# A home of its own for the last batch's turned x2 tiles, and vector and pool work reordered in the second token mixing

## The reference

```python
# layer 1: attention without softmax, then an RMS norm
kv = einsum('bhsd,bhse->bhde', k, v); out = einsum('bhsd,bhde->bhse', q, kv)
x = out / sqrt(mean(out*out) + 1e-6) * g_norm
# layer 2 (w_tok_r, w_tok_i: 576x576; w_theta, w_ch: 512x512)
theta = x @ w_theta
y = einsum('ts,bsd->btd', w_tok_r, x*cos(theta)) + einsum('ts,bsd->btd', w_tok_i, x*sin(theta))
u = x + y; x2 = u + maximum(u @ w_ch, 0)
# layer 3 (w_tok1: 576x256, w_tok2: 256x576, w_ch1: 512x1536, w_ch2: 1536x512)
h = maximum(x2.T @ w_tok1, 0) @ w_tok2        # token mixing, the stage changed
u2 = x2 + h.T
out = u2 + maximum(u2 @ w_ch1, 0) @ w_ch2
```

## Time and profile before

| | before |
|---|---|
| median of the runs | 1263.39 us (1263.16 to 1264.73) |
| time of the profiled execution | 1261.56 us |
| its span, first to last instruction | 1259.7 us |
| mean granted TensorE clock | 0.984 |
| PE busy | 1195.4 us, 95% |
| DVE, ACT, POOL busy | 817.6, 503.4, 367.7 us |

### The profile page before, as it was taken

How to read it: one execution, slowest core, us unless ns; L and a number is a source line. 1 busy time by engine, 2 the same in 40 slices (tenths; PEclk the granted TensorE clock), 3 DMA queues, 4 the chain that set the end, 5 groups by cost and what they waited for, 6 DMA issues and landing times.

```text
span 1259.7 us, 20594 instructions
## 1 busy us (share of the span) xinstructions
PE 1195.4 (95%) x7590; PEld 1157.5 (92%) x7590; DVE 817.6 (65%) x1220; ACT 503.4 (40%) x796; POOL 367.7 (29%) x216
## 2 busy tenths in 40 slices
PE   6999999999999999987789999999999889999998
PEld 5899999999899999987777999999999889999998
DVE  3866767676767666764465566767675676666664
ACT  3533324242524333331333345555566443333331
POOL 4443435444442535240462132133022320000000
PEclk9999999999999999999889999999999999999999
DMA  9924444362715430327768487757649999999982
GB/s 256 172 40 99 76 103 84 77 111 37 149 38 111 71 80 0 76 78 229 228 219 302 158 306 294 259 228 269 254 196 346 348 326 297 257 256 286 275 200 51
DMA packets 348428, 228.12 MB, mean 181 GB/s; under 512 B 268880, under 2 KB 316368, under 8 KB 347344
## 3 DMA queue, kind: packets, MB, share of 16 engines
q1 hardware_dynamic: 348368, 227.32, 62.8%
HBM read 136.84 MB, written 92.80 MB: 182 GB/s over the span
## 4 chain that ended last, share of the span: by engine, by line
PE 61%; issue 14%; DVE 8%; POOL 5%; SPq 4%; DMA 4%; ACT 3%; DVEq 0%; POOLq 0%; ACTq 0%
PE bank L42 11%; PE bank L44 10%; PE bank L43 10%; PE bank L1196 9%; PE bank L1198 9%; PE bank L1197 9%; PE bank L252 2%; DVE weights_fraction L621 1%; POOL z_z L797 1%; SPq L154 1%; DVE tokens_cos L618 1%; DMA weights_down<-w_scratch 1%; SPq L179 1%; PE bank L240 1%; POOL z_z L799 1%
## 5 line engine op out<-in xcount | busy, mean ns | idle before, releaser
L42 PE MATMUL bank<-weights_tok,z_z 128*128 128x288 f32 x576 | 175.3, 304 | 14.7 <-ACT z_z L471 9.2
L43 PE MATMUL bank<-weights_tok,z_z 128*128 128x288 f32 x576 | 171.0, 297 | 0.0
L44 PE MATMUL bank<-weights_tok,z_z 128*128 128x288 f32 x576 | 170.9, 297 | 0.0
L42 PEld LDWEIGHTS bank<-weights_tok,z_z 128*128 128x128 f32 x576 | 109.4, 190 | 18.1 <-ACT z_z L471 10.6
L43 PEld LDWEIGHTS bank<-weights_tok,z_z 128*128 128x128 f32 x576 | 109.6, 190 | 0.0
L44 PEld LDWEIGHTS bank<-weights_tok,z_z 128*128 128x128 f32 x576 | 109.3, 190 | 0.0
L782 POOL TENSOR_TENSOR weights_rms_inverse<-weights_mean_squares,weights_minus_half 128x8 f32<-128x8 f32 x40 | 65.5, 1637 | 136.9 <-DVE weights_mean_squares L588 136.7
L797 POOL TENSOR_TENSOR z_z<-tokens_cos,z_z 128x512 fp32r<-128x512 f32 x32 | 51.3, 1604 | 177.8 <-ACT z_z L471 177.0
L478 ACT ACTIVATE weights_x_channel_major<-attention_u 128x288 fp32r<-128x288 f32 x64 | 28.4, 444 | 150.9 <-DVE attention_u L650 150.9
L42 PE MATMUL bank<-weights_x_channel_major,weights_ch 128*128 128x288 f32 x256 | 77.2, 301 | 0.0
L43 PE MATMUL bank<-weights_x_channel_major,weights_ch 128*128 128x288 f32 x256 | 75.4, 294 | 0.0
(11 more groups left out here) (271 smaller groups left out, 3700.3 us busy)
## 6 DMA issues: line engine op xcount, KB each, us to landing
g_scratch<-attention_staged SPq DMA_DIRECT2D x36, 960.0 KB, 4.7
weights_g<-g_scratch SPq DMA_DIRECT2D x24, 1152.0 KB, 8.4
g_scratch<-attention_staged SPq DMA_DIRECT2D x36, 384.0 KB, 4.7
x_scratch<-attention_u SPq DMA_DIRECT2D x8, 1152.0 KB, 4.5
x_tokens_scratch<-z_x_turned SPq DMA_DIRECT2D x128, 72.0 KB, 2.0
u_scratch<-attention_u SPq DMA_DIRECT2D x8, 1152.0 KB, 7.9
weights_raw_u<-u_scratch SPq DMA_DIRECT2D x6, 1536.0 KB, 9.1
qkv_u_left<-u_scratch SPq DMA_DIRECT2D x12, 768.0 KB, 9.8
```

What stands on the lines that cost most here:

```text
L42: eng.matmul(out, w[0], x[0], start=first, stop=False)
L43: eng.matmul(out, w[0], x[1], start=False, stop=False)
L44: return eng.matmul(out, w[1], x[0], start=False, stop=last)
```

## The change

Three edits, all about phase B.

1. The last batch's turned tiles get tiles of their own, `x2_turned_last`, behind `x2_first_tokens` in region `weights`. `turn_x2` and `store` take the tiles as an argument. ACT's wait for `prev["turned"]` moves from ahead of all its phase-B work to ahead of the first `up_hi`, which writes into region `weights`; POOL's own wait for it goes.
2. DVE's order in each batch: the two `hidden_lo` first, and then the three `x_lo` pieces ahead of residuals 0, 2 and 4.
3. POOL forms the sum `up_sum` before the third `up_lo`, not after it.

```diff
-    turned = m["x2_turned"]
+    turned, turned_last = m["x2_turned"], m["x2_turned_last"]
...
-        store(B - 1)
+        store(B - 1, turned_last)
...
-                    turn_x2(b, g - NC - 1)
+                    turn_x2(b, g - NC - 1, turned if more else turned_last)
...
-        act.wait_ge(*prev["turned"])
...
             if n == 0:
                 act.wait_ge(d_xlo, NPX)
+                act.wait_ge(*prev["turned"])
...
         def batch(n, i, pair, more=True):
-            if more:
-                x_lo(dve, n + 1, 0)
             for mt in range(NM):
                 hidden_lo(n, mt)
-            if more:
-                for piece in range(1, NPX):
-                    x_lo(dve, n + 1, piece)
             for g in range(NG):
+                if more and g % 2 == 0 and g // 2 < NPX:
+                    x_lo(dve, n + 1, g // 2)
                 residual(n, i, pair, g)
...
-        for step in range(3):
+        for step in range(2):
             up_lo(step)
         gp.wait_ge(s_up[2], DMA)
-        gp.wait_ge(*prev["turned"])
         add(up_sum, a11, a21, ALU.subtract)
+        up_lo(2)
         up_lo(3)
...
-                        [("x2_first_tokens", [P, NT, DM], F32)],
+                        [("x2_first_tokens", [P, NT, DM], F32), ("x2_turned_last", [P, 2, S], F32),
+                         ("x2_turned_last", [P, 2, S], F32)],
```

More of the change, by code:

```diff
@@ L166, in load_q, with store @@
                 load_tile(qin, q, n, j, s_q)
-        def store(n):
+        def store(n, tiles=turned):
             wait(sp, d_x2, NG * (n + 1))
@@ L171, in store, with store_turned @@
             for c in range(NC):
-                store_turned(n, c)
-        def store_turned(n, c):
+                store_turned(n, c, tiles[c // 2])
+        def store_turned(n, c, tile):
             sp.wait_ge(d_turned, NC * n + c + 1)
@@ L179, in store_turned @@
                 sp.dma_start(x2t_dram[n, :, first:first + SIDE].rearrange("(b s) d -> s b d", s=SIDE),
-                             turned[c // 2][part * SIDE:(part + 1) * SIDE, c % 2, :].rearrange("p (b d) -> p b d", d=SIDE)
+                             tile[part * SIDE:(part + 1) * SIDE, c % 2, :].rearrange("p (b d) -> p b d", d=SIDE)
                              ).then_inc(s_turned, DMA)
@@ L664, in relu_add, with turn_x2 @@
                                      op0=ALU.max, op1=ALU.add).then_inc(d_x2, 1)
-        def turn_x2(b, c):
+        def turn_x2(b, c, tiles):
             dve.wait_ge(d_x2, NG * b + NC + c + 1)
@@ L672, in turn_x2 @@
                 dve.wait_ge(p_tok, NG * (b + 1))
-            dve.transpose(turned[c // 2][:, c % 2, :], u[:, c, :]).then_inc(d_turned, 1)
+            dve.transpose(tiles[c // 2][:, c % 2, :], u[:, c, :]).then_inc(d_turned, 1)
         def tok_weight_lo(i):
@@ L770, in body @@
                     x_lo(b + 1, j)
-            turn_x2(b, NC - 1)
+            turn_x2(b, NC - 1, turned if more else turned_last)
         body(0, first=True)
```

## The result

The changed kernel takes 1283.03 us (median of 4 runs, 1280.04 to 1284.26), the kernel before 1263.28 us in the same comparison: a ratio of 1.0153, 95% interval 1.013 to 1.0176. It is 19.8 us slower. The forecast was 1279.

A forecast was written before the change was run, and what follows sets the result against it. PE, busy 95%, was taken as the bound, with phase B's one-buffer tokens loop nearly as long as its floor. The start, intervals and POOL turns put the last `mix` 15.9 us later: 1279 us, range 1264 to 1288.

The forecast's parts named there:

- The start, -9.8 us: Phase B's first `mix`: own tiles free ACT, DVE's plain x2 store wait comes next; 596.4, 9.8 us earlier.
- The first interval, 18.2: From `mix(0)` to `mix(1)`: batch 2's tokens, behind two raw weight quarters, come at 612.2; 18.2 us, 14.3 before.
- The loop, 16.2 us without POOL: Tokens' buffer, per batch: 7.2 issue to use, 2.4 to `mix`, 6.6 to next issue; exceeds PE's 12.8 by 3.4.
- the 1.5 for the low clock of the first `mix`: `mix(0)` starting on the low clock delays batch 2's token issue; between nothing and 2.4 us, 1.5 taken.
- POOL against DVE, 5.0 us in batches 1 to 3: `x_lo` 1 waits 2.3 us and `x_lo` 2 2.7 us for whole POOL instructions; batch 4 has one wait, 2.3.
- The last two intervals: The end of phase B: 16.2 us for the loop without POOL, then 12.8 us, PE's own work.
- The sum: Phase B's last `mix` at 725.7 us against 709.8, 15.9 us later; profiled execution 1277.5, median 1279.
- A slowdown by a factor of 2.8: Other reading of stretched `x_lo`: slower while POOL runs, 2.2 us at seven meetings, 15.4 us against the lock's 17.3.
- Only the loop: Rival: phase B's loop lengthens without turns between POOL and DVE; 1262 to 1274 us, chance 0.15.
- the rival of a lesser start: Rival: another wait holds `mix(0)` near 603; up to 6 us over the forecast, 1285, chance 0.12.
- The hidden loop: Rival: phase B's later tokens' load is still in time, as ACT needs it after PE's `hidden`; 1252, chance 0.08.
- POOL's sum first: Ahead of the third `mix`: removes ACT's 7.09 us wait for `up_sum` and PE's 4.72 us stall.

The follow-up runs named there:

- e1: The kernel before with the new DVE order alone; 1293.15 us, ratio 1.0228.
- e2: The changed kernel with the DVE order of before, own tiles and POOL's sum first kept; 1256.93 us, ratio 0.9946 to the kernel before.
- e6: The changed kernel with POOL's `up_lo` of steps 2 to 6 waiting for the last `x_lo` of the same batch; 1273.61 us.
- e7: The changed kernel with 24 matmuls that nobody reads ahead of `mix` in batches 0 to 6; 1277.02 us.
- e4: The kernel before with POOL's sum ahead of the third `up_lo` alone; 1262.65 us, ratio 0.9986.
- e3: The kernel before with the own tiles and the moved ACT wait alone; 1256.96 us, ratio 0.9947.
- e5: The changed kernel, but DVE does all `x_lo` after `hidden_lo` and ahead of all residuals; 1270.27 us, ratio 1.0045 to the kernel before.
- e12: The changed kernel with all `x_lo` ahead of residuals, POOL waiting for the last `x_lo`, and batch 2's tokens issued ahead of two raw quarters; 1251.49 us.

## Why the prediction was right

*The start, -9.8 us.* Right: 599.30 - 589.80 = 9.5 us after the phase's first matmul, against 19.4 before: -9.9. DVE was released by the plain x2 store, as predicted (598.46).

*The first interval, 18.2.* It was 20.1. The tokens were issued 8.1 us after `mix`, as worked out. They took 9.6 us to use and not 7.7. Of these 1.9 us 1.2 are the raw quarters ahead of them, issued 16.0 and not 14.8 us into the phase, as the 16 stores of the turned tiles took 15.6 us to issue and not 14.5; the rest is open.

*The loop, 16.2 us without POOL.* Its terms hold: 2.4 from tokens to `mix` in every batch, 6.7 to 7.4 from issue to use. That 2.4 and the 1.5 for the low clock of the first `mix` (4.65 against 3.15 us to the first residual) came out to the tenth is luck: each was picked between two bounds that no row narrowed. Where POOL has no work the interval was 17.0 (batch 5): 1.3 more for the half clock, 0.5 less for the load. e1 and e2 show that the DVE order alone makes the loss, e6 that the turns with POOL are a part of it. The part of the clock is read from rows and not isolated by a run.

*POOL against DVE, 5.0 us in batches 1 to 3.* The sum was nearly right, its parts were not. I had two meetings per batch, 2.3 and 2.7 us, and no clock. There was one, `x_lo` 2, for 2.5 us, and half clock for 2.0 (5.2 against 3.15 to the first residual): 4.5 in all. But the two are not independent. What sets the interval is when POOL's second instruction ends, and this I had at 10.9 us after `mix`; it was 10.55 (650.26 - 639.71). Until then a slow clock and a wait for POOL exchange one for one, which is the reason I gave for leaving the clock out, and e7 bears it out: on the full clock there were two meetings and the interval was no shorter. In batch 4 I had one meeting of 2.3 us; there it was 0.2 (1.42 instead of 1.22) and the half clock 1.8, again an exchange: 18.2 against 18.5.

*The last two intervals.* 16.2 and 12.8 were forecast, 17.0 and 14.1 came: a pause of 2.74 us ahead of batch 6 was enough for a first matmul at 0.58 us there, 1.3 us that the sum did not have.

*The sum.* Phase B: 15.9 later by the forecast, 17.9 by the trace (730.63 - 589.80 against 709.80 - 586.82). The medians say 19.8. The errors are +1.9 in the first interval, -2.0 in the next four and +2.1 in the last two. Two of them cancel, and that the total is as near as 4 us to the forecast is luck to this extent; the loop that outgrew PE's work is not.

The Trainium skill, page "SBUF — State Buffer", section "Who interferes with whom", says that a vector instruction with at most one SBUF input, outside the 2-port modes, does not contend with GpSimd, and that one with two contends with a GpSimd instruction that reads SBUF. The trace agrees: two residuals at 644.94 took 0.82 us with POOL's `up_lo` running to 645.72, while the `x_lo` at 647.65 stood until POOL's next one ended. A slowdown by a factor of 2.8, the other reading that the prediction weighed, does not fit: that `x_lo` took 4.6 times its 0.69 us, and the one at 645.67, which came first, its usual 1.22, while POOL's sum beside it took 4.58 instead of 3.4.

*The rivals.* "Only the loop" is nearly what e6 makes: 1273.6, at the upper edge of the 1262 to 1274 that it was given. Nothing held `mix(0)` near 603, so the rival of a lesser start is out. The hidden loop did not come about in any kernel with residuals ahead of the last `x_lo`. That POOL's sum first would free 4.72 us was too much: alone it is worth 0.5 to 3 us (e4), beside the tiles nothing (e2 against e3).

## What to carry to other kernels

When a single buffer is refilled by a load of some microseconds, the instruction that frees it belongs ahead of everything that is merely due soon; add up the loop (land, split, free, issue, land) and compare it with the work that has to hide it, before moving anything in front of that instruction. Two delays that end at the same event, here a slow clock and a wait for POOL, are not added: the later one counts. Where two engines take turns by whole instructions, an order that misses a long instruction by 0.1 us is not a safe order: make the off-path engine wait explicitly. And before taking a transfer off the path, write down the next loop through the same queue, here the store's, as it may be longer.

## What the runs showed of the hardware that was not expected

A DVE instruction of 0.69 us (64 partitions, 512 elements, both inputs in SBUF) costs up to 3.9 us next to POOL instructions of 3.5 us, and the wait falls on whichever comes second, even by 0.1 us (e5). It is seen as a longer instruction and not as idle time, so a table of waits does not show it.

PE's clock does not follow from the length of the last pause alone. In the changed kernel the first matmul of `mix` took 0.58 us, half clock, after pauses of 2.74 to 5.93 us; but after one of 2.87 us (599.30) it took 0.37, and the slow matmuls of 0.44 began 0.8 us later. In e12 the `mix` after a pause of 3.25 us (613.04) ran on the full clock until a second pause inside it. With 24 unread matmuls in the pause the clock read 1.00 in the window of `mix(2)` instead of 0.56, and the interval stayed as it was.
